# One fp32 kernel of attention, routed experts and a cosine layer: another order of the first head, split late rows, quarter pieces in the last layer

## The reference

```python
# attention: q, k, v are (2, 8, 1152, 64); q is averaged in pairs of rows, so 576 queries a head
q_pool = q.reshape(B, H, S // 2, 2, D).mean(axis=3)
attn = softmax(q_pool @ k.T / sqrt(D)) @ v
x = attn.transpose(0, 2, 1, 3).reshape(1152, 512)          # 1152 tokens
# routed experts: 8 experts, the two best of each token
noisy = x @ w_gate + log1p(exp(x @ w_noise)) * noise
top2, w = the two largest of noisy, and their softmax
x = sum over the two experts e of w_e * (relu(x @ w1[e]) @ w2[e])   # 512 -> 1024 -> 512
# last layer
h = x @ w_in                                               # 512 -> 2048
out = (h * cos(h)) @ w_out                                 # 2048 -> 512
```

## Time and profile before

| | us |
|---|---|
| median of three runs (lowest, highest) | 850.01 (848.75, 851.17) |
| the profiled execution | 848.37 |
| its span, first to last instruction | 846.7 |
| TensorE busy | 834.7 |
| VectorE busy | 508.0 |
| ScalarE busy | 415.3 |
| GpSimd busy | 402.6 |

### The profile page before, as it was taken

One profiled execution on the slowest core, in us unless ns is written; L12 is line 12 of the kernel. 1 busy time (PEld: TensorE's weight loads), 2 busy tenths in 40 slices (PEclk: granted clock), 3 DMA queues, 4 the chain that ended last, 5 costly groups with the idle time before them and its releaser, 6 DMA issues.

```text
span 846.7 us, 15351 instructions
## 1 busy us (share of the span) xinstructions
PE 834.7 (99%) x4858; PEld 743.9 (88%) x4859; DVE 508.0 (60%) x994; ACT 415.3 (49%) x762; POOL 402.6 (48%) x293
## 2 busy tenths in 40 slices
PE   7999999999999999999999999999999999999998
PEld 6899999999999897888887888888888889999997
DVE  6888878888888886332322222232366775676564
ACT  3777777777777774211211111121145665565554
POOL 7664445556887005548879959568432030000000
PEclk9999999999999999999999999999999999999999
DMA  4212111142242016987645635353444021000100
GB/s 118 82 43 74 54 42 42 42 143 84 91 144 75 1 57 223 285 313 230 221 157 186 198 136 198 136 196 138 134 143 133 1 75 37 2 0 1 38 1 37
DMA packets 51520, 91.27 MB, mean 108 GB/s; under 512 B 9376, under 2 KB 18592, under 8 KB 50976
## 3 DMA queue, kind: packets, MB, share of 16 engines
q1 hardware_dynamic: 40832, 67.26, 23.9%
q0 software_dynamic: 3360, 11.01, 4.5%
q10 hardware_dynamic: 7296, 12.59, 4.5%
HBM read 73.78 MB, written 17.06 MB: 107 GB/s over the span
## 4 chain that ended last, share of the span: by engine, by line
PE 91%; DVE 4%; ACT 2%; POOL 2%; issue 1%; DMA 0%; POOLq 0%; DVEq 0%; ACTq 0%
PE ps L1676 10%; PE ps L1678 10%; PE ps L1677 10%; PE ps L1491 5%; PE ps L1524 5%; PE ps L1540 5%; PE ps L1542 4%; PE ps L1541 4%; PE ps L1525 4%; PE ps L1803 4%; PE ps L1802 4%; PE ps L1801 4%; PE ps L1788 3%; PE ps L1786 3%; PE ps L1787 3%; PE ps L1482 3%
## 5 line engine op out<-in xcount | busy, mean ns | idle before, releaser
L639 POOL TENSOR_TENSOR W<-stage,W 128x2048 fp32r<-128x2048 f32 x32 | 147.2, 4601 | 2.6
L1035 DVE TENSOR_REDUCE mx<-ps 128x1 f32<-128x384 f32 x225 | 121.6, 551 | 10.1 <-PE ps L1491 8.6
L793 ACT ACTIVATE ph<-ps 128x576 fp32r<-128x576 f32 x144 | 93.7, 651 | 66.3 <-PE ps L1525 65.9
L1053 DVE TENSOR_TENSOR pl__80<-ps,ph 128x576 fp32r<-128x576 f32 x144 | 107.9, 750 | 14.0 <-ACT ps L800 13.8
L800 ACT ACTIVATE ps<-ps 128x576 f32<-128x576 f32 x144 | 93.6, 650 | 0.0
L1540 PE MATMUL ps<-ph,vs 128*65 128x288 f32 x288 | 86.2, 299 | 0.5 <-ACT ot L747 0.5
L873 ACT CAST hh<-ps 128x512 fp32r<-128x512 f32 x50 | 26.9, 590 | 120.5 <-PE ps L1715 120.5
L1542 PE MATMUL ps<-ph,vs 128*65 128x288 f32 x288 | 84.8, 294 | 0.0
L1524 PE MATMUL ps<-qat,kt 128*128 128x288 f32 x288 | 83.8, 306 | 0.9 <-ACT qbt L740 0.6
L1541 PE MATMUL ps<-pl__80,vs 128*65 128x288 f32 x288 | 84.6, 294 | 0.0
L1676 PE MATMUL ps<-W,xh 128*128 (+1 forms) x200 | 80.1, 400 | 1.2 <-POOL W L639 0.7
(11 more groups left out here) (221 smaller groups left out, 1960.7 us busy)
## 6 DMA issues: line engine op xcount, KB each, us to landing
stage<-in_moe_w_dram SPq DMA_DIRECT2D x32, 1024.0 KB
y_slots<-ys ACTq DMA_DIRECT2D x25, 256.0 KB
x_slots<-ring SPq DMA_DIRECT2D x22, 256.0 KB
xs<-x_slots ACTq DMA_DIRECT2D x22, 256.0 KB
kn<-in_k_dram SPq DMA_DIRECT2D x16, 288.0 KB, 3.3
vn<-in_v_dram SPq DMA_DIRECT2D x16, 288.0 KB, 2.9
stage<-in_moe_w_in_dram SPq DMA_DIRECT2D x4, 1024.0 KB
stage<-in_moe_w_out_dram SPq DMA_DIRECT2D x4, 1024.0 KB
```

Of the source, the lines that this page charges most:

```text
L639: pl.tensor_tensor(W[:, slot, 1, part], stage[:, j % 2, :], W[:, slot, 0, part].bitcast(F32), ALU.subtract).then_inc(w_ready, 1)
L1035: ve.tensor_reduce(mx3[:, i:i + 1], ps[:, bank_of(hh, ("m", i)), 0:PIECE], AX_X, ALU.max).then_inc(m_ev, 1)
L1053: ve.tensor_tensor(pl_[:, j % 3, :].rearrange("p (a n) -> p a n", a=2), ps[:, 2 * s_par(hh, j):2 * s_par(hh, j) + 2, 0:HQ], ph[:, j % 3, : ...
```

## The change

In the first head the rounding of k and one copy of q move from VectorE to ScalarE, the second k bank's copy from ScalarE to VectorE, and the query bank is copied in two pieces, of which the first maxima wait for the first only. The low queries' padding is filled at the start. After the maxima TensorE turns the low queries of the first four tiles first, then the second head's tail and its k banks, and the waits for fills, gate weights and the turning matrix are taken apart. Before the table stand four matmuls on old data instead of two. A late tile is split into high and low parts, scaled with the slot's gate, and multiplied by a matrix of zeros and ones: eight one-pass matmuls instead of four fp32 ones. The last layer's first two groups are interleaved; the second half of w_out is split in eight pieces of 512 columns at groups 1 to 8, ahead of the sine on ScalarE and ahead of the product on VectorE; and the first low part of the activation is made one instruction earlier.

```diff
-HALF = 1024
+QUARTER = 512
-X2_BANKS = (0, 1, 4, 6)
+X2_BANKS = (0, 1, 6, 7)
...
# ScalarE, first head
-            for slot in (("n", 0), ("n", 1), TAIL, ("n", 3)):
-                kq_move(0, 0, slot, FIRST_BANK[slot])
-            kq_move(0, 1, ("n", 0), 0)
-            kq_move(0, 1, ("n", 1), 1)
+            act.wait_ge(k_in[0], 16)
+            sc.copy(ks[:, 0, :, 0, :].bitcast(F32R), kn[:, 0, :, :]).then_inc(kh_done, 1)
+            act.wait_ge(qp_done, 1)
+            sc.copy(qa[:, :, 1, :].bitcast(F32R), qp[:, :, :]).then_inc(qa_done, 1)
+            act.wait_ge(kq_done, 1)
+            sc.copy(kt[:, 0, 0:BANK], ps[:, FIRST_BANK["n", 0], :]).then_inc(first_ev, 1)
+            act.wait_ge(kq_done, 3)
+            sc.copy(kt[:, 0, 2 * BANK:S], ps[:, FIRST_BANK[TAIL], P:2 * P]).then_inc(first_ev, 1)
+            act.wait_ge(kq_done, 4)
+            sc.copy(qat[:, 0, 0:P], ps[:, FIRST_BANK["n", 3], 0:P]).then_inc(first_ev, 1)
+            sc.copy(qat[:, 0, P:4 * P], ps[:, FIRST_BANK["n", 3], P:4 * P])
+            act.wait_ge(n1_ev, 1)
+            sc.copy(qat[:, 0, 4 * P:QW], ps[:, FIRST_BANK[TAIL], 2 * P:3 * P]).then_inc(kq_ev, 4)
             qb_move(0, 0, 0)
+            kq_move(0, 1, ("n", 0), 0, turned=2)
             qb_move(0, 0, 1)
-            kq_move(0, 1, TAIL, bank_of(0, ("q", 1)))
+            kq_move(0, 1, ("n", 1), 5, turned=3)
+            kq_move(0, 1, TAIL, bank_of(0, ("q", 1)), turned=1)
...
+            def late_high(k):
+                act.wait_ge(y_done, LATE + k + 2)
+                act.wait_ge(late_done, k + 1)
+                at_least(act, late_read, k)
+                sc.activation(ysh[:, :], ps[:, 5, :], ACT.Copy, scale=late_gate[:, k:k + 1]).then_inc(late_hi, 1)
...
# ScalarE, last layer (low_quarter on VectorE likewise, behind low_g and before the wait for the cosine)
                 if g > 0:
                     high_g(g - 1, (f - 1) % F2C)
+                if blk == 0 and 1 <= f <= 8:
+                    high_quarter(f - 1)
                 cos_of(g)
-                if blk == 0 and 2 <= f < 6:
-                    high_half(f - 2)
...
# VectorE
+            dve.wait_ge(kq_done, 2)
+            ve.tensor_copy(kt[:, 0, BANK:2 * BANK], ps[:, FIRST_BANK["n", 1], :]).then_inc(n1_ev, 1)
...
-                then(ve.tensor_tensor(late_sel[:, k, :], late_n[:, 0, :], late_n[:, 1, :], ALU.add))
+                then(ve.tensor_tensor(late_sum[:, :], late_n[:, 0, :], late_n[:, 1, :], ALU.add))
+                ve.tensor_scalar(late_hot[:, k, :], late_sum[:, :], 0.0, None, ALU.is_gt)
+                ve.tensor_reduce(late_gate[:, k:k + 1], late_sum[:, :], AX_X, ALU.add).then_inc(late_done, 1)
+                dve.wait_ge(late_done, k + 1)
+            def late_low(k):
+                dve.wait_ge(late_hi, k + 1)
+                at_least(dve, late_read, k)
+                ve.scalar_tensor_tensor(ysl[:, :], ps[:, 5, :], late_gate[:, k:k + 1], ysh[:, :].bitcast(F32),
+                                        ALU.mult, ALU.subtract).then_inc(late_lo, 1)
...
+                if left <= 1:
+                    late_low(1 - left)
                 move_y(t)
...
                 dve.wait_ge(t1_red, g + 1)
+                if g == 1:
+                    low_g(0, 0)
...
# TensorE
-            pe.wait_ge(kq_ev, 4)
+            pe.wait_ge(n1_ev, 1)
+            pe.wait_ge(first_ev, 3)
             for c in range(QC):
                 at_least(pe, m0_ev, c - 1)
+                if c == 1:
+                    pe.wait_ge(kq_ev, 4)
...
-            for i in range(2):
-                kq_group(0, 1, ("n", i), i)
-            pe.wait_ge(zeroed, FILLS - 2)
-            qb_group(0, 0, 0)
+            pe.wait_ge(kq_ready, 2)
+            pe.wait_ge(m0_ev, 4)
+            low_queries(0, 0, 0)
             kq_group(0, 1, TAIL, bank_of(0, ("q", 1)))
-            qb_group(0, 0, 1)
-            pe.wait_ge(zeroed, FILLS)
+            kq_group(0, 1, ("n", 0), 0)
+            qb_group(0, 0, 1, start=True)
+            kq_group(0, 1, ("n", 1), 5)
             pe.wait_ge(k1_filled, 2)
+            cycle(0, 1, True, True, False, False, start=True)
             pe.wait_ge(gate_in, 64)
-            cycle(0, 1, True, True, False, False, start=True)
+            pe.wait_ge(turner_done, 1)
...
-            warm(WARM_R // 2)
+            warm(WARM_R)
...
             def late_rows(k):
-                pe.wait_ge(y_ev, LATE + k + 1)
+                pe.wait_ge(late_hi, k + 1)
                 for c in range(DC):
-                    last = pe.matmul(ps[:, X2_BANKS[c], 0:BLK], ys[:, c * P:(c + 1) * P], late_sel[:, k, :],
-                                     start=(k == 0), stop=(k == 1))
+                    pe.matmul(ps[:, X2_BANKS[c], 0:BLK], ysh[:, c * P:(c + 1) * P], late_hot[:, k, :],
+                              start=(k == 0), stop=False)
+                pe.wait_ge(late_lo, k + 1)
+                for c in range(DC):
+                    last = pe.matmul(ps[:, X2_BANKS[c], 0:BLK], ysl[:, c * P:(c + 1) * P], late_hot[:, k, :],
+                                     start=False, stop=(k == 1))
...
+            def first_pair():
+                # high_part(g, c): w high and w low by fh; low_part(g, c): w high by fl
+                for c in range(DC):
+                    pe.wait_ge(bh_ev, c + 1)
+                    high_part(0, c)
+                    if c < 2:
+                        high_part(1, c)
+                    pe.wait_ge(bl_ev, c + 1)
+                    last = low_part(0, c)
+                last.then_inc(h2_done, 1)
+                for c in range(DC):
+                    if c >= 2:
+                        high_part(1, c)
+                    last = low_part(1, c)
+                last.then_inc(h2_done, 1)
```

96 lines of the change are left out of this document (60 added, 36 removed).

## The result

The changed kernel takes 844.33 us (median of five runs, 843.83 to 844.89) against 850.01 us for the kernel before, run beside it (five runs, 847.70 to 852.41). The ratio is 0.9934, 95% interval 0.9911 to 0.9957: 5.68 us less, 3.7 to 7.6 us by the interval. The direction was right, and so was the mechanism of the largest term, the last layer's first block.

What follows compares the result with a forecast made beforehand. TensorE, busy 834.7 of 846.7 us, was taken as the bound. Terms -0.4 + 0.05 - 0.1 - (1.85 + 0.4) gave -2.7 us, 845.7 us profiled; with 1.64 us to the median 847.3 us, range 845.4 to 849.6 us.

Steps and rivals of the forecast that it cites:

- the last layer's first block: Weight quarters in the activation chain's gaps: steps near 3.3 us, 1.85 us gained by the sixth group, 0.4 us at the eleventh.
- the last line of the sum: From profiled run to median: the median lies 1.64 us above the profiled run, so 845.7 us becomes 847.3 us.
- the first head: First head: query turns first bring scores 0.44 us sooner, 0.4 us taken; nothing counted for maxima starting 0.3 us sooner.
- first rival: Late rows pay more, first tile up to 1.1 us and chain 0.5 us sooner: 845.8 us, chance 0.15.
- upper bound of 0.8 us: First head: most it could gain, if the early 0.3 us of the maxima comes through as well.
- The table: Two more matmuls ahead of the table fill a wait for VectorE: 0.05 us lost (0.3 lost to 0.1 gained).
- The late rows: Two late tiles: split matmuls save 1.29 us each if fed; VectorE's queue leaves the first tile 0.1 us.
- the second tile: Second late tile, before the last layer: TensorE gains 0.4 us, the activation chain loses 0.3 us.
- the early first low part: Last layer: low part of the first activation ahead of one reduction, output group 0 starts 0.5 us sooner by this.
- the wait between the high and the low late rows: Late rows: a TensorE wait between high and low matmuls, named as a sign, no size given.
- the second (the head gives nothing): First head gives nothing, as GpSimd's end and the next copy set the start: 847.7 us, chance 0.13.
- third and fourth rivals: Third: quarters don't fit, 848.4 us, chance 0.12; fourth: both quarters exposed in full, step 4.53 us, 851.1 us, chance 0.10.

Runs made afterwards that it cites:

- e2_loop: Kernel before with only the last layer's first block changed (eight quarters in the gaps, first low part earlier): 847.35 us, ratio 0.9974.
- e15_head_warm: Kernel before with the first-head edit and four matmuls on old data ahead of the table: 846.79 us, ratio 0.9969.
- e1_head: Kernel before with only the first-head edit: 847.34 us, ratio 0.9979.
- e7_all_oldhead: Changed kernel with the old first head put back: 846.26 us, ratio 0.9974.
- e5: The changed kernel run again, beside the kernel before: 845.05 us, ratio 0.9957.
- e4_warm: Kernel before with only four matmuls on old data ahead of the table instead of two: 848.66 us, ratio 1.0002.
- e6_all_warm2: Changed kernel with two matmuls on old data ahead of the table instead of four: 844.62 us, ratio 0.9948.
- e3_late: Kernel before with only the late rows split and the last layer's first two groups interleaved: 848.71 us, ratio 1.0001.
- e8_all_oldlate: Changed kernel with the old fp32 late rows and no interleaved first pair: 845.02 us, ratio 0.9957.
- e13_head_loop: Kernel before with the edits of e1_head and e2_loop together: 844.33 us, ratio 0.9947.
- e14_head_halves: Kernel before with the first-head edit, the early first low part and four uncut weight halves moved into the gaps: 844.41 us, ratio 0.9948.
- e11_halves_in_gap: Kernel before with the four weight halves moved into the activation step's gaps, not cut in quarters: 847.02 us, ratio 0.9971.
- e12_fill: Kernel before with eight more matmuls on old data in two gaps of the first head: 849.21 us, ratio 0.9991.
- e9_early: Kernel before with only the first head's opening changed (split over two engines, first maxima on 128 query columns): 848.12 us, ratio 0.9984.
- e10_reorder: Kernel before with only the first head's order behind the maxima changed: 848.77 us, ratio 0.9990.

## Why the prediction was wrong, step by step

**Two steps failed.** The measured median lies 3.0 us under the forecast of 847.3 us. The larger part, 2.2 us, is the last line of the sum: the median was taken to lie 1.64 us above the profiled run after the change too, and it lies 0.56 us below it (844.33 and 844.89 us). The smaller part, 0.8 us, is in the sum itself, where 845.7 us was worked out for the profiled run; the first head makes it, with 0.4 us forecast and 1.47 us in the traces, of which the expert stretch took 0.4 us back. With 1.47 us there the forecast would still have been 846.2 us. That the first rival's 845.8 us lies nearer to the measured time is luck, as its mechanism did not come.

**The first head.** It had three pieces. (1) "I count nothing for" the earlier maxima, because GpSimd's split was taken to hold TensorE at 15.60 us and the maxima's end was called "near that point already". This is the piece that failed. In the old order that wait holds the k tiles; behind them the query turns wait for the fifth maximum, at 16.59 us in the earlier trace rows. The rows of the kernel before:

```profile
14.67 0.88 POOL L617 TENSOR_TENSOR qb<-qp,qa 128x320 f32<-128x320 f32 x1 [0.17 <-POOL ks L612]
...
16.70 0.42 PEld L1499 LDWEIGHTS ps<-ident,qb 128*128 128x128 f32 x4 [0.24 <-issue]
```

The row that ended with a POOL wait was an early one of two, and I took it for the last. In this one execution it nearly was: the split alone would have let the scores start at about 18.2 us (15.55 + 2.64 us), 0.1 us before they did. In the five other profiles with the distance of 1.70 to 1.71 us the same sum lies 0.2 to 1.3 us before the scores (2.6 us in e2_loop with its late clock), so there the maxima decided clearly. (2) The order behind the turns: 2.25 us forecast, 2.24 us measured, and 2.25 us in e15_head_warm too. Right in size. (3) GpSimd's end at 15.55 us was taken as a constant. It is not: the split starts between 8.60 and 10.11 us over the profiled executions of all kernels, in most of them when q has landed, and the profile of before had the latest start of them all.

How much the head is worth. The 1.47 us of the profiled pair are in part a draw, of the landing and of the clock's rise. The new head has its scores at 16.73 to 17.64 us in eight profiles (median 17.04 us), the old head at 17.70 to 18.39 us in the six whose full clock had come by 8.3 us (median 17.90 us): 0.86 us. Of these 0.4 us are the earlier maxima (medians of their start 9.41 and 9.78 us), for which 0.3 us had been seen and nothing counted, and the rest is the order, 0.44 us by the forecast. Paired runs put the head edit at 1.8 us alone (e1_head) and 1.2 us beside the rest (e7 against e5), and at a clock of 1.00 at 1.7 us (846.26 us in five executions of e1_head against 847.95 us) and 0.6 us. So it is worth 0.6 to 1.8 us; 0.4 us was too low, while the prediction's upper bound of 0.8 us, "if the early 0.3 us comes through as well", fits the profiles' 0.86 us.

**The table.** Right: +0.05 forecast, nothing found (e4_warm, e6_all_warm2).

**The late rows.** Right for the first tile, in mechanism and size: 0.1 us forecast and 0.09 us in the trace, and the wait for VectorE's second sum stands where it was put. On the second tile I gave TensorE 0.4 us and took 0.3 us from the chain. TensorE got 0.02 us, as ScalarE's bank copies are held by the store's issue and TensorE waits 0.60 us for them; the chain lost 0.45 us. The stretch from the last product to the first output group is 0.10 us shorter all the same, 0.2 us by the forecast, as the early first low part pays for it: the stretch is 17.96 us in e3_late, which has the late rows without it, 17.4 to 17.5 us in the four profiles with both, 17.5 us in the three with it alone, and 17.5 to 17.65 us in the seven with neither. So the 0.5 us that it was to bring by itself is not there. Nor is the wait between the high and the low late rows that was named as a sign: the low ones start 0.80 us behind the high ones, which take 0.70 us by their pitch. e3_late and e8_all_oldlate confirm that the late rows bring nothing. The first rival (the late rows pay more) is refuted, the second (the head gives nothing) too.

**The last layer's first block.** Right: 3.3 us a step with a quarter, both waits of 0.41 us gone, 1.66 us against 1.65 us up to the sixth group and 0.49 against 0.4 us up to the eleventh. The third and fourth rivals are refuted by the step of 3.26 us. The gain is the same in all profiles with the loop's edit: 20.9 to 21.0 us against 22.6 to 22.7 us, and 22.22 us against 22.7 us for the next five groups. A quarter on VectorE measures 0.68 us; by the Trainium skill, "VectorE: DVE Perf Modes", section "The TRN2 errata", its formula gives 0.69 us, and the trace agrees within 0.01 us. Its advice against small tiles is true of the busy time, 8 x 0.68 us against 4 x 1.22 us, and costs nothing here, since e13_head_loop and e14_head_halves take the same time: an idle gap pays for it. The scaled high part of a late row took 0.69 us where I had taken 0.70; "ScalarE: Activation LUTs" of the Trainium skill, section "What ACT_TABLE_LOAD costs", gives 186 + 0.833 x 512 + 93 ns = 0.71 us with one pointer operand, and the trace agrees within 0.02 us.

**From the profile to the median.** The forecast carried a difference from the profiled run over to a median of three runs. That median was high: over 92 later runs beside the experiments the kernel before has 849.15 us. Of these, 26 ran at a granted clock of 1.00 with a median of 847.95 us and 60 at 0.998 or less with 849.35 us. Of 35 runs of kernels that hold the new head and the new last-layer loop (the changed kernel twice, e6, e8, e13, e14), 29 ran at 1.00 with 844.38 us and 6 at 0.998 with 845.74 us. So at an equal clock the gain is 3.6 us in both groups (847.95 - 844.38 and 849.35 - 845.74), near the 3.56 us of the profiled pair. About 2.15 us are the loop's by its two stretches; the other 1.4 us are the head's and what can't be placed, as the profiles give the head 0.86 us. The other 2.1 us of the 5.68 us are what 850.01 us lies above 847.95 us: up to 1.4 us for a fall of the clock, which most executions of the kernel before have (60 of 92) and few of the new ones (6 of 35), and at least 0.7 us by which its first few runs came out high. How many of those had a fall is not on record, so this division is an estimate. The five runs of the changed kernel in that comparison had no fall.

**What stays open.** Why the falls are rarer. They were seen in 5 of 11 executions of e1_head, 5 of 7 of e2_loop, 6 of 12 of e3_late, 10 of 12 of e11, 3 of 10 of e7_all_oldhead, but 2 of 12 of e4_warm and 1 of 7 of e15_head_warm, and in none of 6 of e6_all_warm2. Neither the head's gaps (e12_fill) nor one part alone explains this. With head and loop the two added matmuls ahead of the table are not needed for it (3 of 18 executions of e6, e13 and e14, which leave them out, had a fall). Without the loop they go with few falls as well (3 of 19 executions of e4_warm and e15_head_warm, against 30 of 42 of the kernel before beside them); by what way, no run shows. How the head's gain divides between opening and order stays open too: e9_early and e10_reorder lie too near the noise, and the medians of profiles are of few executions.

## What to carry to other kernels

Before a wait in the profile is called the gate, follow the engine's own order one step on: where two waits stand one behind the other (here GpSimd's split, then the fifth maximum), what ends the second one decides, and its distance to the next stage, alike in several executions, shows it. Then ask by how much: here the two gates were 0.1 us apart in the profile read and up to 1.3 us in others with an ordinary clock. A median that lies above the profiled run is a draw too, and is no term to carry over to another kernel without its own range: here it made 2.2 us of the 3.0 us. The landing time of a DMA in one profile is one draw; a term that rests on it needs a range from it, about 1.5 us here. And work that lengthens a chain belongs in the gaps that the chain itself shows: its place was worth 2.2 us and its size nothing.

## What the runs showed of the hardware

- The granted clock falls to half for about 3 us in many executions, with a mean of 0.998 or less in 60 of 92 executions of the kernel before on three chips; in the profiled e2_loop at 24.7 us and at 325.1 us, in e11_halves_in_gap at 319.9 us. TensorE had been busy 4.82 of 5.00 us before the one at 325.1 us; during it the 512-column matmuls of the first expert tile start 0.43 us apart (325.61 to 327.75 us) instead of 0.23 us.
- The trace's record of the full clock begins at 5.3 to 8.3 us in most profiled executions (e1_head's has no record) and at 14.5 and 13.4 us in two of them, e2_loop and e10_reorder, whose maxima therefore started at 11.4 us instead of 8.9 to 10.3 us.
- The changed kernel spent 287.7 us from the first tile of the expert loop to the last expert product in one profiled execution and 286.9 us in the other, at a granted clock of 1.00 in both; the kernel before has 287.0 us. A difference of 0.3 us in this stretch, as in the table at the top, can't be told from chance.
